# Attention with float32 exponentials in place in PSUM, and both units of transposed scores ahead of the next pair's second unit of scores

## The reference, cut to what matters

```python
def _attn_ref(q, k, v):                      # (4, 8, 576, 64) each
    scores = scale * np.matmul(q, k.transpose(0, 1, 3, 2))
    mask = (rel >= 0) & (rel < 128)          # rel = query position - key position
    scores = np.where(mask, scores + bias[None], -1000000000.0)
    scores = scores - np.max(scores, axis=-1, keepdims=True)
    attn = np.exp(scores)
    attn = attn / (np.sum(attn, axis=-1, keepdims=True) + 1e-09)
    return np.matmul(attn, v)

def _moe_ref(x, w_ch1, w_ch2):               # x is (4, 576, 512)
    u = x + np.real(np.fft.fft(np.fft.fft(x, axis=1), axis=2))
    un = (u - mean(u)) / np.sqrt(var(u) + 1e-06)
    return u + np.maximum(un @ w_ch1, 0.0) @ w_ch2
```

## Time and profile before

| | us |
|---|---|
| median of 3 runs | 1095.93 |
| the runs | 1095.2, 1101.27, 1095.93 |
| time of the profiled execution | 1102.07 |
| span of its profile | 1100.2 |
| attention (22.86 to 244.17) | 221.31 |
| spectrum (244.17 to 308.92) | 64.75 |
| PE busy, share of the span | 89% |
| DVE, ACT, POOL busy | 44%, 31%, 27% |

### The profile page before, as it was taken

How to read it: one execution, slowest core, us unless ns; L and a number is a source line. 1 busy time by engine, 2 the same in 40 slices (tenths; PEclk the granted TensorE clock), 3 DMA queues, 4 the chain that set the end, 5 groups by cost and what they waited for, 6 DMA issues and landing times.

```text
span 1100.2 us, 21125 instructions
## 1 busy us (share of the span) xinstructions
PE 984.0 (89%) x8090; PEld 628.6 (57%) x8091; DVE 486.8 (44%) x902; ACT 345.3 (31%) x456; POOL 294.0 (27%) x249
## 2 busy tenths in 40 slices
PE   3878888889969999999999999991599999999995
PEld 1545555557757667676776777651355555555552
DVE  3777767744443243333424333546876488000000
ACT  2445545541111111121111111110144554554551
POOL 0345544550011010010101100000355455554531
PEclk9888888889989999999999999995699999999998
DMA  6233333322220110101101110430554466111100
GB/s 244 69 97 112 111 102 111 90 90 77 69 72 21 39 39 19 57 19 38 38 19 38 38 38 6 135 104 7 177 187 144 155 205 217 37 42 50 38 18 1
DMA packets 50668, 87.18 MB, mean 79 GB/s; under 512 B 6052, under 2 KB 21491, under 8 KB 50365
## 3 DMA queue, kind: packets, MB, share of 16 engines
q1 hardware_dynamic: 45181, 70.52, 20.6%
q0 software_dynamic: 5440, 16.00, 4.5%
HBM read 71.78 MB, written 16.55 MB: 80 GB/s over the span
## 4 chain that ended last, share of the span: by engine, by line
PE 81%; DVE 10%; ACT 4%; issue 2%; DMA 2%; POOL 1%; DVEq 0%; SPq 0%; ACTq 0%; POOLq 0%
PE psum L724 17%; PE psum L739 17%; PE psum L825 12%; PE psum L849 12%; PE psum L653 6%; PE psum L681 2%; PE psum L838 2%; PE psum L566 2%; DVE arena L1120 2%; PE psum L591 2%; DVE m_mem L1116 2%; PE psum L573 2%; PE psum L535 1%; DVE m_mem L1099 1%; ACT arena L901 1%
## 5 line engine op out<-in xcount | busy, mean ns | idle before, releaser
L724 PE MATMUL psum<-m_mem,arena 128*128 (+1 forms) x1728 | 201.2, 275 | 2.0 <-DVE m_mem L1265 2.0
L739 PE MATMUL psum<-arena,m_mem 128*128 128x512 f16 x864 | 195.3, 379 | 0.0
L724 PEld LDWEIGHTS psum<-m_mem,arena 128*128 128x128 f16 x1728 | 169.5, 98 | 29.1 <-DVE m_mem L1265 2.4
L825 PE MATMUL psum<-arena,m_mem 128*128 x600 | 136.8, 385 | 1.4 <-ACT m_mem L1020 1.4
L849 PE MATMUL psum<-arena,m_mem 128*128 x600 | 135.3, 382 | 2.3 <-ACT m_mem L1034 2.3
L739 PEld LDWEIGHTS psum<-arena,m_mem 128*128 128x128 f16 x864 | 84.5, 98 | 90.4
L973 ACT ACTIVATE m_mem<-psum 128x512 f16<-128x512 f32 x72 | 43.0, 597 | 264.6 <-PE psum L724 264.6
L1454 POOL TENSOR_TENSOR arena<-arena 128x1024 f16<-128x1024 f32 x32 | 69.9, 2183 | 138.0 <-ACT arena L901 138.0
L1270 DVE SCALAR_TENSOR_TENSOR m_mem<-psum,m_mem 128x512 f16<-128x512 f32 x72 | 49.8, 692 | 119.1 <-ACT m_mem L973 119.1
L825 PEld LDWEIGHTS psum<-arena,m_mem 128*128 128x128 f16 x600 | 58.6, 99 | 68.8 <-issue 5.8
L849 PEld LDWEIGHTS psum<-arena,m_mem 128*128 128x128 f16 x600 | 58.1, 98 | 68.8 <-issue 4.7
(11 more groups left out here) (182 smaller groups left out, 1208.3 us busy)
## 6 DMA issues: line engine op xcount, KB each, us to landing
dimdft_sb<-in_exp_w SPq DMA_DIRECT2D x74, 256.0 KB
wstage<-in_exp_w SPq DMA_DIRECT2D x54, 256.0 KB, 3.1
m_mem<-in_qk SPq DMA_DIRECT2D x16, 576.0 KB, 4.8
wstage<-in_mlp_w SPq DMA_DIRECT2D x32, 256.0 KB, 2.7
m_mem<-in_v SPq DMA_DIRECT2D x32, 160.0 KB, 4.3
x_rows<-m_mem SPq DMA_DIRECT2D x16, 320.0 KB, 2.9
x_rows<-m_mem SPq DMA_DIRECT2D x9, 512.0 KB, 2.8
m_mem<-in_seq_dft SPq DMA_DIRECT2D x1, 1440.0 KB, 9.0
```

The source lines that it names most:

```text
L724: last = nc.tensor.matmul(psum[:, 2 + k % 4, (f % 2) * 2 * P:(f % 2 + 1) * 2 * P], w1_sb[:, sp_, c, f * P:(f + 1) * P], unT[:, bass.ds(t % ...
L739: last = nc.tensor.matmul(psum[:, 6 + q, :], hT[:, k % 4, sp_, at:at + P], w2_sb[:, mp, f, :], start=f == 0 and sp_ == 0 and mp == 0, stop ...
L825: last = nc.tensor.matmul(psum[:, 2 + half, :], xeT[:, sp_, c, :], slots[:, bass.ds(slot, 1), at:at + 512] .rearrange("p o n -> p (o n)"), ...
```

## The change

1. **Exponentials.** ACT writes the high parts first and then the float32 exponentials over the scores in PSUM, in place. DVE subtracts out of PSUM (`p_lo_of`), POOL no longer does. `scores_t` of the next pair waits for that subtraction (`p_lo`) and not for `p_hi`. The buffer `p32` is gone, and the third buffer of q and k lies in its place.
2. **PE's order.** Both transposed units stand ahead of the next pair's second unit of scores, probabilities times v is one step per head (`pv(p - 1, 0)` and `pv(p - 1, 1)`), both for the pair before, and `max_to_row` is last.
3. **PE's matmuls.** In the units the bias of both heads is added in one run of wider matmuls (up to 512 columns), and the maxima are selected by matmuls over one head's 64 partitions, side by side for the two heads.
4. **v.** POOL scales v in place (`v_scale`), ACT makes the high part from that, POOL subtracts for the low part. DVE no longer does.
5. **Normalisation** is one step per pair.
6. **Weights.** No chunk is split in attention. All 32 are split in the spectrum, two per quarter, the high part on ACT and the low part on DVE, from six staging buffers, four of them in the space of q and k. The loops of ACT and DVE over the batches are unrolled.
7. Semaphores are split or joined accordingly; the setup on DVE makes the selection matrix in three passes, for which ACT doesn't wait.

```diff
             def scores_t(p, u):
...
                 if p > 0:
-                    pe.wait_ge(p_hi[u], p)
+                    pe.wait_ge(p_lo[u], p)
...
+                if u == 1:
+                    bias(True, False)
+                for c in ((0, 1), (2, 3, 4))[u]:
+                    col = CPLACE[c][1]
+                    products(parts, at, CKEYS[c], (col, col + CQUERIES[c]), 1, c * P, 0, c * P, c == 0)
+                last = less_max(u == 1)
+                if u == 0:
+                    last = bias(False, True)
                 last.then_inc(st_ready[u], 1)
...
                 scores_t(p, 0)
                 if more:
                     scores(p + 1, 0)
-                if p > 0:
-                    pv_high(p - 1, 0)
+                scores_t(p, 1)
                 if more:
                     scores(p + 1, 1)
-                scores_t(p, 1)
+                if p > 0:
+                    pv(p - 1, 0)
                 if more:
                     scores(p + 1, 2)
-                pv_low(p)
+                if p > 0:
+                    pv(p - 1, 1)
                 if more:
                     max_to_row(p + 1)
-                if p > 0:
-                    pv_high(p - 1, 1)
...
             def exp_of(p, u):
                 act.wait_ge(st_ready[u], p + 1)
-                if p > 0:
-                    act.wait_ge(p_lo[u], p)
-                nc.scalar.activation(p32[:, u], psum[:, 2 + 2 * u:4 + 2 * u, :], ACT.Exp, bias=exp_shift,
-                                     scale=SSCALE)
                 if p > 1:
-                    act.wait_ge(pv_done[1], p - 1)
-                nc.scalar.activation(ptparts[:, p % 2, u, 0], psum[:, 2 + 2 * u:4 + 2 * u, :], ACT.Exp,
-                                     bias=exp_shift, scale=SSCALE).then_inc(p_hi[u], 1)
+                    act.wait_ge(pv_done, p - 1)
+                bank = psum[:, 2 + 2 * u:4 + 2 * u, :]
+                nc.scalar.activation(ptparts[:, p % 2, u, 0], bank, ACT.Exp, bias=exp_shift, scale=SSCALE)
+                nc.scalar.activation(bank, bank, ACT.Exp, bias=exp_shift, scale=SSCALE).then_inc(p_hi[u], 1)
...
             def v_hi_of(p, a):
-                act.wait_ge(v_loaded[a], 16 * p + 16)
+                act.wait_ge(v_scaled, 2 * p + a + 1)
...
+            def p_lo_of(p, u):
+                dve.wait_ge(p_hi[u], p + 1)
+                nc.vector.tensor_tensor(ptparts[:, p % 2, u, 1], psum[:, 2 + 2 * u:4 + 2 * u, :], ptparts[:, p % 2, u, 0],
+                                        ALU.subtract).then_inc(p_lo[u], 1)
...
                 more = p + 1 < PAIRS
+                if p > 0:
+                    p_lo_of(p - 1, 1)
                 if p > 1:
-                    normalise(p - 2, 1)
-                for a in range(2):
-                    v_lo_of(p, a)
+                    normalise(p - 2)
                 if more:
                     max_of(p + 1, 0)
+                p_lo_of(p, 0)
+                if more:
+                    max_of(p + 1, 1)
+                    max_of(p + 1, 2)
+                    neg_of(p + 1)
                 if p + 2 < PAIRS:
                     qk_lo_of(p + 2)
...
+            def v_scale(p, a):
+                pool.wait_ge(v_loaded[a], 16 * p + 16)
+                nc.gpsimd.tensor_scalar(v_sb[:, a], v_sb[:, a], XS, None, ALU.mult).then_inc(v_scaled, 1)
...
             for p in range(PAIRS):
-                p_lo_of(p, 0)
+                for a in range(2):
+                    v_scale(p, a)
                 if p > 1:
                     x_lo_of(p - 2)
-                p_lo_of(p, 1)
+                for a in range(2):
+                    v_lo_of(p, a)
...
+            def w_hi_of(n):
+                act.wait_ge(w_loaded[n % RING], 16 * (n // RING + 1))
+                nc.scalar.activation(wparts[:, 0, n * CH:(n + 1) * CH], w_staging[n % RING], ACT.Copy, scale=WS)\
+                    .then_inc(w_hi, 1)
...
             def spectrum_lo(b):
...
-                    w_hi_of(PAIRS + DC * b + c, c % 2, 16 * (2 * b + c // 2 + 1 + (PAIRS if c % 2 == 0 else 0)))
-                    w_lo_of(PAIRS + DC * b + c, c % 2)
+                    for n in range(2 * (DC * b + c), 2 * (DC * b + c) + 2):
+                        w_lo_of(n)
```

More of the change, by code:

```diff
@@ L522, in _, with twice, products @@
             THREE = ((0, 0), (0, 1), (1, 0))
+            def twice(ap):
+                return ap.unsqueeze(1).to_broadcast([ap.shape[0], 2, ap.shape[1]])
+            def products(parts, banks, rows, cols, mine, m0, other, o0, first, last=False):
+                for i, (mine_lo, other_lo) in enumerate(THREE):
+                    for a in range(2):
+                        half = parts[a * DH:(a + 1) * DH]
+                        done = nc.tensor.matmul(psum[0:rows, banks + a, cols[0]:cols[1]], half[:, mine_lo, mine, m0:m0 + rows],
+                                                half[:, other_lo, other, o0:o0 + cols[1] - cols[0]],
+                                                start=first and i == 0, stop=last and i == 2)
+                return done
             def scores(p, j):
@@ new lines, in less_max @@
+                def less_max(last):
+                    for t, lo, hi in (((0, 0, P), (1, P, 3 * P), (2, 3 * P, 4 * P)),
+                                      ((2, 0, P), (3, P, 3 * P), (4, 3 * P, 4 * P)))[u]:
+                        for a in range(2):
+                            rows = slice(a * DH, (a + 1) * DH)
+                            o = psum[:, at + a, lo:hi]
+                            m = max_row[rows, 0:SROWS[t]]
+                            if hi - lo > SROWS[t]:
+                                o = o.rearrange("p (n q) -> p n q", n=2)
+                                m = twice(m)
+                            done = nc.tensor.matmul(o, rowsel_sb[rows, t, :], m, start=False, stop=last and t == 4)
+                    return done
@@ L946, in spectrum_hi @@
                                          ACT.Copy).then_inc(uhi_done, 1)
-            with act.Fori(0, B) as b:
+                    for n in range(2 * (DC * b + c) + 2, 2 * (DC * b + c) + 4):
+                        if n < WCH:
+                            w_hi_of(n)
+            for n in range(2):
+                w_hi_of(n)
+            for b in range(B):
                 spectrum_hi(b)
@@ L1205, in _ @@
                                            op0=ALU.mult, op1=ALU.subtract).then_inc(wg_split, 1)
-            with dve.Fori(0, B) as b:
+            for b in range(B):
                 spectrum_lo(b)
@@ L1497, in _ @@
             pool.wait_ge(const_in, 5 * 16)
-            pool.wait_ge(x_stored, 16 * PAIRS)
+            for par in range(2):
+                pool.wait_ge(x_stored[par], 16 * PAIRS // 2)
             gather_x(0, first=True)
```

293 lines of the change are left out of this document (129 added, 164 removed).

## The result

| | before | after |
|---|---|---|
| median of 3 runs, us | 1095.93 (1095.2 to 1101.27) | 1056.42 (1053.62 to 1057.44) |
| profiled execution, own time and span, us | 1102.07, 1100.2 | 1057.44, 1055.6 |
| mean granted clock, profiled execution | 0.943 | 0.955 |
| first transposed scores to the spectrum's first matmul, us | 221.3 | 176.8 |
| from there to line 681 before, line 700 after, us | 64.75 | 64.97 |

The ratio of the times is 0.962, with a 95% interval of 0.957 to 0.968. The two profiled executions lie 44.6 us apart, and nearly all of that is attention: 44.5 us less there, 0.6 less ahead of it, 0.2 more in the spectrum. Its sum for a profiled execution was 1056 us, against 1057.44.

The account below looks back on a forecast made before the run. Attention was taken as bound by PE in order, stretched by DVE's stalls behind POOL and the slow clock. Profiled 1102.07 - 46 - 0.3 + 0.3 = 1056 us, median less 46 = 1050; forecast the middle, 1053, range 1036 to 1081.

Parts of the forecast that it names:

- The ring: Attention: v's load, scaling, high part, exponentials, q and k, x high, x low, v's low parts, handoffs: 10.9 us a pair.
- Exponential into PSUM: ACT in attention: taken at 1.11 us like the PSUM to SBUF one, between 1.0 and 1.3.
- PE's loop: PE in attention: 8.9 us of matmuls, 0.6 for the stop at the maxima, small waits: 9.9 us a pair.
- The shared port: DVE beside POOL: PSUM subtractions not lengthened; the ten-element subtraction of the maxima held up to 0.8 us, not 2.
- The clock full but for the first pairs: PE in attention: longest stand about 1 us; the clock fell behind stands of 2.5, so 1.0 from the fourth pair.
- a dear and a cheap kind: Attention before the change: one pair of 15.73 us at clock 0.78, the next, same work, 11.79 us at 1.00.
- Spectrum +0.3: Spectrum: all 32 weight chunks hidden by PE; DVE's last job, ahead of the clearing PE waits for, 0.3 us longer.
- The choice of 1053: Whole kernel: the middle between 1056 us, from the profiled execution, and 1050, the median less 46.
- (b): Attention: loads of 2.1 and scaling of 0.3 us, PE's loop of 9.9 binds; 1036 us, chance 0.13.
- (c): Attention: v lands in 4.3 us, 12.7 us a pair, and the clock falls; 1081 us, chance 0.17.
- (d): Spectrum: ACT waits for a weight chunk, 1 us in each of 16 quarters; 1069 us, chance 0.06.
- (e): Attention: POOL's small instructions cost 1.4 us each, x low 2.5, load 4.3, 16 us a pair; 1131 us, chance 0.04.

Follow-up runs that it names:

- e2: The kernel after with four buffers of v in place of two, so v is loaded a pair earlier: 1045.34 us.
- e7: The kernel after with four buffers of v and, on POOL, v's low parts made ahead of x's: 1036.84 us.
- e1: The kernel after with POOL making v's two low parts ahead of x's low part: 1042.51 us.
- e4: The kernel after with the score units' matmuls back in the old sequence, maxima still half-height pairs: 1060.63 us.
- e3: The kernel before with one wait added, so POOL's second 1024-wide subtraction of a pair cannot start ahead of line 1116: 1072.79 us.
- e8: e7 with the spectrum's first quarter of batch 0 put ahead of the last pair's value matmuls: median of 4 runs 1031.46 us.
- e5: e2 with the score units' matmuls in the old sequence, as in e4: 1058.35 us.

## Why the prediction was right, step by step

**The ring binds, at 10.9 us a pair: right, 10.82.** The chain shows it, and the runs bear it out from two sides. Opening the ring shortens the pair (9.76 in e2, 9.46 in e7; in e1, which opens it in part, most pairs are 9.5 to 10.3); 1.0 us more on PE or a fill of 1.06 us on DVE does not lengthen it. PE's work was 8.88 us against the forecast's 8.9. ACT's own terms add up to 7.25 us and not to the 7.4 that the forecast wrote; it was 6.89.

**The terms of the ring: two mis-sized and two misplaced, and the errors cancelled.** The forecast closed the ring through one load (2.5), one scaling (0.6), and two low parts (1.6), 4.7 us. It really goes through the first head's load (2.20), both scalings (2.1 with the gap between them) and the first head's low part alone (0.75), 5.1 us. The load was well read: 2.2 to 2.4 for 160 KB, and that the 4.3 of the earlier trace rows was the time behind q and k is borne out by e1, where the load stands right behind them again and takes 4.5. The scaling was not. It takes 1.01 us where the bounds were 0.2 and 0.8. The forecast took the subtraction of the same width as the upper end, and the scaling is dearer than it (0.75 to 0.78). The handoffs came to 0.3 us, where 0.4 were counted, and the high parts of v and x cost the chain 0.16 us less than their full durations. The forecast also wrote 2.1 us for the two exponentials and 1.1 for q and k, where its rows give 2.2 and 1.16; in the chain they take 2.08 and 1.08, since each starts a little ahead of the end of the one before. That the sum of all this came out at 10.9 is in part luck. For the scaling the upper bound should have been the nearest row with a margin, since nothing in the trace said that one input is cheaper than two.

**Exponential into PSUM** 1.11, between 1.0 and 1.3: 1.086. **Subtraction out of PSUM** 1.22: 1.221. **Normalisation of 640** 0.82: 0.825. A line through two widths of the same form was good to 0.01 us.

**PE's loop 9.9: close.** It can't be seen in the kernel after, where the ring covers it. With four buffers it is 9.76, and with the cast free of POOL as well 9.46.

**The shared port: the right price at the wrong instruction.** The forecast gave the ten-element subtraction up to 0.8 us. It is the cast one line earlier that is held, 0.56 us as the median where 0.176 is its time; the subtraction behind it is free at 0.17. The forecast had cleared every instruction with fewer than two SBUF inputs, and the cast has one. The Trainium skill (SBUF — State Buffer, "Who interferes with whom") clears such an instruction only outside the modes in which it uses both ports, a condition that the forecast left out, and it lists cast among the instructions that can enter such a mode, and so contend with GpSimd. The trace agrees: the cast ends with POOL's instruction (119.33 and 119.31). In the kernel after the ring hides this; with the ring open the pair of e2 is 0.30 us longer than that of e7, and the cast in it takes 0.42 us instead of 0.18, so it has the larger share.

**The clock full but for the first pairs: partly wrong.** The mean of attention is 0.93, not near 1. It was down at 34 us, again from 64 to 71 us, and from 194 us at the end of the stage to 203 in the spectrum. The step that failed is that only stands of 2.5 us bring it down. Ahead of 64 us PE had stood 1.41 and then 0.48 us, and in e4 it fell behind stands of 0.25, 0.29 and 0.37 us, in the part of a pair that has the narrow 64-row matmuls. The distances show the cost as about 1.0 us for each such pair: 11.83 at 64 us where 10.8 is usual. The size of it: 16 pairs of 10.82 would be 173.1 us, and attention took 176.8, so the ends and the slow clock cost 3.7 us, for which the forecast had 1. That is the mis-sized term; the pairs, 0.08 us each under the forecast, gave 1.3 of it back.

**How the old pairs were read.** The forecast took 15.73 and 11.79 as a dear and a cheap kind that take turns. Counted from copy to copy the distances are mostly 13.76 us (one is 15.13 and one 15.75), and twice 13.76 is the sum of its two. PE stands 2.49 us for line 1116 at the end of every other pair (106.37, 133.89) and 0.56 us at the end of those between (92.65, 120.17). So one of two pairs has the stand and the next has the slow clock: PE is busy 10.38 us in the one and 12.41 in the other, for the same 164 matmuls. The forecast's cuts put both into one stretch. The mean that went into the sum, 13.83, was measured over the whole stage and holds either way, and e3, where the meeting alone is removed, gives the 11.80.

**Spectrum +0.3: the number right, not by its path**, +0.2. The 32 chunks there are hidden: PE is busy 64.56 of 64.97 us, and the one gap is 0.41 us ahead of line 700. The forecast's +0.3 was to come from DVE's last job ahead of that line, but the wait there was 0.47 us before, so it did not grow. PE itself was busy 0.28 us longer, and the slow clock at the start of the stage lasted longer too, until about 203.7 us (4.7 us of it), where it was until about 248.2 (4.1 us of it) before. That the two numbers agree is luck. The same holds ahead of attention, -0.3 expected and -0.6 measured: in the traces of e1, e2 and e4 to e8, whose setup is that of the kernel after or nearly so, attention begins anywhere from 21.70 to 22.95 us.

**The choice of 1053: the weaker half of the arithmetic.** The sum for the profiled execution (1056) was 1.4 us from what was measured. The forecast then went to the middle between it and the median less 46, on the belief that 1102.07 was unusual. Seven more runs of the kernel before, on another chip, lie between 1096.48 and 1101.22, with median 1098.55. So the profiled one was not far out, if chips can be compared to 3 us, which is not shown.

**The rivals.** (b), the ring short and PE's loop binding, came true only where the ring was opened by an edit; its 1036 us is what e7 took (1036.84). (c) fell with the load of 2.4 us in the kernel after; its load of 4.3 came back in e1, by a swap in POOL's order alone. (d) fell in the spectrum, where it had PE wait 1 us in each quarter. (e) had POOL's small instructions at 1.4 us each (it names four, and its ring of 16 us holds three); they are 1.01 and 0.78, and x's low part is back at its minimum of 1.40 (2.51 as a rule in the earlier trace rows).

**Where the 44.5 us came from**, per pair at full clock: 11.80 (e3, port meeting gone) to 10.69 (e5, the change with its old matmul sequence and the ring open) to 9.76 (new sequence) is what the change could have given, and the ring takes 1.06 back, for 10.82. The first of these steps, 1.1 us, mixes the order of the units, the exponentials in place, the maxima as half-height pairs, v on POOL, the single normalisation and the weights gone from the stage; these were not tried apart. What the ring costs is from e2 against the kernel after, 1045.34 against 1056.42, 11 us, with one run of e2 on a chip of its group; the ring and the cast's meeting together are 20 us, from e7 at 1036.84.

Still open: why POOL's scaling of one input (1.01 us) is slower than its subtraction of two (0.78). It wasn't tried with another output type or out of place. And why the clock falls in one pair and not in the next with nearly the same stands.

## What to carry to other kernels

When a step moves to another engine, follow its buffer all the way round: done, load, every engine in its program order, done again. Add that ring up against each engine's own sum; with one buffer per item it may bind while every engine has slack, and then work saved on an engine outside the ring buys nothing. A second buffer or a swap of two steps in one engine's order is the cheap cure (11 and 14 us here, 20 together). Look then where the swap moves the load: here it went right behind a larger one and took 4.5 us instead of 2.4. Independent work of the next stage fills the stand at the end of a pipeline and keeps the clock up (5 us). And before a large rewrite, see whether one tiny instruction on the critical path is held by another engine: a single wait in the code brought 27 us of attention, where the rewrite brought 44.

## What the runs showed of the hardware that was not expected

- POOL's multiplication of 128 x 320 float32 by a constant, in place, takes 1.01 us, and its two-input subtraction of the same size with a float16 result 0.775.
- A cast of ten elements on DVE, with one SBUF input, is held by POOL's subtraction, for up to 0.72 us instead of 0.176. And POOL is held as well: two scalings took 2.85 us behind DVE's low part of q and k.
- The granted clock fell to 1.2 GHz behind PE stands of 1.41 and 0.48 us (the kernel after, 64 us) and of 0.25, 0.29 and 0.37 us (e4, 101 us) with narrow matmuls between them, not only behind 2.5 us. In most pairs of both kernels such stands did not bring it down, so they are not shown to be the whole cause.
- A load of 160 KB lands 2.4 us after its issue in the kernel after, where it goes out 5.75 us behind one of 576 KB, and 4.5 us after it in e1, where it goes out 1.16 us behind.
- An exponential of 1024 elements from PSUM to PSUM takes 1.086 us, one from PSUM to SBUF 1.106, in the same pairs.
